# Attention with a top-32 mask, then two expert layers: transposes and v products moved seven and eight heads behind the scores

## The reference, cut to what matters

```python
# attention: B=2, H=8, S=576, D=64
scores = q @ k.T / 8
mask = scores >= (32nd largest of the row)
attn = softmax(where(mask, scores, -1e9))
x = (attn @ v)                      # rearranged to 1152 tokens x 512
# first expert layer: each token goes to one of 8 experts
e_idx = argmax(x @ w_gate + modality_bias[modality_id]);  gate_w = its probability
x[tokens of e] = gate_w * (relu(x @ w1[e]) @ w2[e])
# second expert layer: all of 4 experts, weighted
out = sum_e p[:, e] * (relu(x @ w1b[e]) @ w2b[e])
```

## Time and profile before

| what | us |
|---|---|
| median of 3 runs | 984.77 (984.18 to 985.72) |
| the profiled execution | 985.48 |
| its span in the profile | 983.7 |
| PE busy | 916.5 (93%) |
| DVE busy | 559.4 (57%) |
| ACT busy | 340.7 (35%) |
| POOL busy | 280.1 (28%) |

### The profile page before, as it was taken

The page is one execution under the profiler, slowest core; times in us unless marked ns, Lnnn a source line. Parts: engine busy times, 40 slices in busy tenths (PEclk is TensorE's granted clock), DMA queues, the critical chain, the costliest instruction groups (busy, mean ns, idle before and its releaser), DMA issues.

```text
span 983.7 us, 13497 instructions
## 1 busy us (share of the span) xinstructions
PE 916.5 (93%) x4849; PEld 770.0 (78%) x4849; DVE 559.4 (57%) x1100; ACT 340.7 (35%) x726; POOL 280.1 (28%) x224
## 2 busy tenths in 40 slices
PE   4799999987799999995699979999999999999998
PEld 4688888876667767762477868998989898989897
DVE  4999999659998989834655152332314231423121
ACT  3545555433445645531645141221202120212010
POOL 7667665434657665611011030000000000000000
PEclk8579999978989999998699989999999999999999
DMA  9120000000412632533962441020202020000001
GB/s 215 57 94 22 1 23 12 12 11 21 173 34 87 214 108 97 187 114 104 330 216 101 152 179 70 1 83 4 86 1 78 9 85 0 0 0 0 32 11 53
DMA packets 49396, 75.63 MB, mean 77 GB/s; under 512 B 24624, under 2 KB 24624, under 8 KB 49328
## 3 DMA queue, kind: packets, MB, share of 16 engines
q1 hardware_dynamic: 42160, 61.09, 18.2%
q0 software_dynamic: 4160, 13.63, 4.3%
q10 hardware_dynamic: 3008, 0.05, 0.2%
HBM read 63.49 MB, written 11.27 MB: 76 GB/s over the span
## 4 chain that ended last, share of the span: by engine, by line
PE 85%; issue 5%; POOL 4%; DVE 4%; DMA 1%; ACT 1%; ACTq 0%; POOLq 0%; DVEq 0%
PE bank L1270 19%; PE bank L1271 18%; PE bank L1272 18%; PE bank L1326 9%; PE bank L1392 5%; PE bank L1367 4%; PE bank L1265 3%; PE bank L1383 3%; PE bank L1297 3%; POOL att L605 2%; PE bank L1295 2%; POOL att L608 1%; DVE w1l L1152 1%; DMA x_tok<-y_a,a_pos_i 1%; PE bank L1338 1%
## 5 line engine op out<-in xcount | busy, mean ns | idle before, releaser
L605 POOL TENSOR_SCALAR att<-sc,top 128x576 f32<-128x576 f32 x70 | 120.8, 1725 | 149.8 <-DVE top L1011 138.0
L1011 DVE MAX8 top<-work 128x8 f32<-128x576 f32 x216 | 152.4, 745 | 0.1
L1270 PE MATMUL bank<-xT,w1h 128*128 128x384 f32 x384 | 129.5, 337 | 5.3 <-DVE w1l L1152 5.3
L1271 PE MATMUL bank<-xT,w1l 128*128 128x384 f32 x384 | 129.1, 336 | 0.0
L1272 PE MATMUL bank<-xT,w1h 128*128 128x384 f32 x384 | 129.0, 336 | 0.0
L1207 DVE SCALAR_TENSOR_TENSOR hT<-bank,hT 128x384 fp32r<-128x384 f32 x96 | 53.0, 557 | 130.8 <-ACT hT L914 127.3
L914 ACT ACTIVATE hT<-bank 128x384 fp32r<-128x384 f32 x96 | 46.9, 492 | 200.9 <-PE bank L1272 200.9
L1326 PE MATMUL bank<-v_one,attT 128*128 128x65 f32 (+3 forms) x800 | 112.8, 282 | 0.6 <-ACT av L738 0.6
L1270 PE MATMUL bank<-w2h,hT 128*128 128x512 f32 x288 | 112.2, 390 | 1.2 <-DVE hT L1207 1.2
L1326 PEld LDWEIGHTS bank<-v_one,attT 128*128 128x128 f32 (+3 forms) x800 | 98.9, 190 | 17.7 <-issue 10.4
L1272 PE MATMUL bank<-w2l,hT 128*128 128x512 f32 x288 | 112.2, 390 | 0.0
(11 more groups left out here) (239 smaller groups left out, 1520.2 us busy)
## 6 DMA issues: line engine op xcount, KB each, us to landing
w_raw<-in_moe_w_dram SPq DMA_DIRECT2D x96, 512.0 KB, 5.9
q_raw<-in_q_dram SPq DMA_DIRECT2D x18, 128.0 KB, 2.7
v_one<-in_v_dram POOLq DMA_DIRECT2D x18, 128.0 KB, 5.5
out_dram<-x_tok SPq DMA_DIRECT2D x9, 256.0 KB, 2.0
k_raw<-in_k_dram SPq DMA_DIRECT2D x8, 256.0 KB, 5.2
y_dram<-zero POOLq DMA_DIRECT2D x2, 1024.0 KB, 6.6
y_dram<-b_ys POOLq DMA_DIRECT2D x7, 256.0 KB
x_dram<-x_cur SPq DMA_DIRECT2D x6, 256.0 KB, 2.8
```

The lines of the kernel that those rows point to most:

```text
L605: nc.gpsimd.tensor_scalar(att[:, g % ATR, :], sc[:, g % RING, :], top8[:, g % RING, 3, 7:8], None, ALU.is_ge).then_inc(keep_made, 1)
L1011: nxt = nc.vector.max(out=top8[:, g % RING, i + 1, :], in_=work[:, j, :])
L1270: nc.tensor.matmul(dst, high_lhs, high_rhs, start=start, stop=False)
L1271: nc.tensor.matmul(dst, low_lhs, high_rhs, start=False, stop=False)
```

## The change

It changes no arithmetic. EXP_LAG, TR_LAG and AV_LAG go from 2, 5, 6 to 3, 7, 8, and `att` gets a fourth slot. `normalise(t)` of tiles 0 to 2 moves from the pair of head 8t + 12 to the pair of head 8t + 10, and their `x_transpose` from step 8t + 17 to 8t + 16; later tiles keep their pair and are transposed in step 8t + 19. `split_q(t + 1)` moves ahead of mask 8t, `round_q` one step earlier. `keep_dense` makes three products instead of four. `ranks`, `sum_tokens` and the first slot stand in steps 34, 37 and 41 instead of 37, 40 and 46, and DVE's chunks of `route` are placed by a finer count. The loop has 82 steps instead of 80.

```diff
-        att = a_mid.take("att", [P, 3, S])
+        att = a_mid.take("att", [P, 4, S])
...
-        RING, EXR, ATR = 8, 4, 3
-        EXP_LAG, TR_LAG, AV_LAG, X_LAG, L_LAG = 2, 5, 6, 17, 18
-        STEPS = (T - 1) * H + AV_LAG + H + 2
-        A_START, A_STEP, SPREAD = 46, 7, 5
+        RING, EXR, ATR = 8, 4, 4
+        EXP_LAG, TR_LAG, AV_LAG = 3, 7, 8
+        STEPS = HEADS + AV_LAG + 2
+        RANKS_AT, TOKENS_AT, A_START, A_STEP, SPREAD = 34, 37, 41, 7, 5
...
+        def x_step(t):
+
+            if t == T - 1:
+                return HEADS + AV_LAG
+            return t * H + (16 if t < GA.tiles else 19)
...
             def beside():
-                yield from clock.until(A_START - 3)
+                yield from clock.until(A_START - 2)
                 pool.wait_ge(x_kept, 16 * TB)
...
             for g in range(HEADS - 2):
+                if g % H == 0 and g // H + 1 < T:
+                    split_q(g // H + 1)
                 mask(g)
...
-                if g % H == 1 and g // H + 1 < T:
-                    split_q(g // H + 1)
...
-                if p % H == 2 and p // H + 1 < T:
+                if p % H == 1 and p // H + 1 < T:
                     round_q(p // H + 1)
...
             def beside():
-                yield from clock.until((GA.tiles - 1) * H + L_LAG + 1)
-                yield from route(GA, clock.until((GA.tiles - 1) * H + L_LAG + 4), clock.until((GA.tiles - 1) * H + L_LAG + 8))
+                yield from clock.until(RANKS_AT - 4.5)
+                yield from route(GA, clock.until(RANKS_AT - 3.4), clock.until(TOKENS_AT - 3.6))
...
-                if g0 >= H + 4 and (g0 - H - 4) % H == 0:
-                    between = normalise((g0 - H - 4) // H)
+                for t in range(T - 1):
+                    if g0 == t * H + (10 if t < GA.tiles else 12):
+                        between = normalise(t)
...
-                for i in range(4):
+                for i in range(3):
                     moving = v_one[0][:, i, 0:KC - 1, :].rearrange("p c w -> p (c w)")
...
-                    if p == (GA.tiles - 1) * H + L_LAG + 3:
+                    if p == RANKS_AT:
                         ranks(GA)
-                    elif p == (GA.tiles - 1) * H + L_LAG + 6:
+                    elif p == TOKENS_AT:
                         sum_tokens(GA)
```

More of the change, by code:

```diff
@@ L219, in q_at, with x_at, logits_at @@
             return t if r == 4 and t < T else None, t if r == 5 and t < T else None
[L221 to L226, removed]
+        def x_step(t):
+            if t == T - 1:
+                return HEADS + AV_LAG
+            return t * H + (16 if t < GA.tiles else 19)
+        def x_at(p):
+            return next((t for t in range(T) if x_step(t) == p), None)
+        def logits_at(p):
+            return x_at(p - 1)
         turn_use = {}
@@ L240, in attention_and_experts @@
                 next_use("ql", low)
[L241 to L244, removed]
+            if x_at(p) is not None:
+                next_use("x", x_at(p))
+            if logits_at(p) is not None:
+                next_use("lg", logits_at(p))
         AV_END = HEADS + AV_LAG - 1
@@ L511, in _ @@
                 clock.now = p
-                if x_at(p, X_LAG) is not None:
-                    keep_x(x_at(p, X_LAG))
+                if x_at(p) is not None:
+                    keep_x(x_at(p))
                 low = q_at(p)[1]
@@ L772, in beside @@
             def beside():
-                yield from clock.until(A_START - 8)
+                yield from clock.until(RANKS_AT + 2)
                 act.wait_ge(GA.lsub_made, 1)
@@ L831, in _ @@
                     read_q(low, "ql", qTl, mixed_l)
-                if x_at(p, X_LAG) is not None:
-                    read_x(x_at(p, X_LAG))
+                if x_at(p) is not None:
+                    read_x(x_at(p))
                 if 0 <= p - TR_LAG < HEADS:
@@ L839, in _ @@
                     key_high(SPLIT - 1 + p)
-                if x_at(p, L_LAG) is not None:
-                    read_logits(x_at(p, L_LAG))
+                if logits_at(p) is not None:
+                    read_logits(logits_at(p))
                 advance(work_beside)
@@ L992, in find_thresholds, with pause @@
                 pair = (g0, g0 + 1)
+                def pause():
+                    advance(work_beside)
+                    clock.now += 1 / 7
+                clock.now = g0
                 for g in pair:
@@ L997, in find_thresholds @@
                     nc.vector.max(out=top8[:, g % RING, 0, :], in_=sc[:, g % RING, :]).then_inc(max_found, 1)
-                    advance(work_beside)
+                    pause()
                 k0 = g0 * 5
@@ L1068, in route @@
                 step(nc.vector.tensor_scalar(g.counts[:, 1, :], g.counts[:, 0, :], 0.0, None, ALU.is_gt))
-                yield
                 step(nc.vector.tensor_tensor(g.cmp_pre[:, :, :, :], below[:, :, :].rearrange("p (o e) f -> p o e f", o=1).broadcast_to([P, 2, E + 1, E]),
@@ L1120, in beside @@
             def beside():
-                yield from clock.until((GA.tiles - 1) * H + L_LAG + 1)
-                yield from route(GA, clock.until((GA.tiles - 1) * H + L_LAG + 4), clock.until((GA.tiles - 1) * H + L_LAG + 8))
+                yield from clock.until(RANKS_AT - 4.5)
+                yield from route(GA, clock.until(RANKS_AT - 3.4), clock.until(TOKENS_AT - 3.6))
             work_beside = beside()
             for g0 in range(0, HEADS, 2):
-                clock.now = g0 + 4
                 between = ()
-                if g0 >= H + 4 and (g0 - H - 4) % H == 0:
-                    between = normalise((g0 - H - 4) // H)
+                for t in range(T - 1):
+                    if g0 == t * H + (10 if t < GA.tiles else 12):
+                        between = normalise(t)
                 find_thresholds(g0, between, work_beside)
@@ L1407, in beside @@
                     else:
-                        keep_dense(MB + 2 if p < (GA.tiles - 1) * H + L_LAG + 6 else MB)
+                        keep_dense(MB + 2 if p < TOKENS_AT else MB)
                 for s in range(SPREAD):
@@ L1510, in _ @@
                     q_transposes(low, "ql")
-                if x_at(p, X_LAG) is not None:
-                    x_transpose(x_at(p, X_LAG))
+                if x_at(p) is not None:
+                    x_transpose(x_at(p))
                 if 2 <= p < 2 + T - 1 - SPLIT:
@@ L1521, in _ @@
                     transpose_att(p - TR_LAG)
-                if x_at(p, L_LAG) is not None:
-                    x_logits(x_at(p, L_LAG))
+                if logits_at(p) is not None:
+                    x_logits(logits_at(p))
                 advance(work_beside)
```

## The result

The changed kernel takes 993.09 us (median of 3 runs, 992.48 to 996.31) against 984.77: ratio 1.0092, 95% interval [1.0056, 1.0128]. It is 8.3 us slower. The forecast was 987.0 with a range of 962 to 1003. The profiled execution took 992.48 us, its span is 990.7 (before 983.7).

A forecast was written before the change was run, and what follows sets the result against it. PE and DVE were taken to march side by side without room, PE slower during the slots. The last v product 11.2 us later, less 9.0 of tail, turned 985.48 into 987.7 profiled, 987.0 median; range 962 to 1003.

The forecast's parts named there:

- Slower, by this mechanism: Tiles 0 to 2: den waits for the v product (5.5, 7.2 us), PE idles for x_cur, then half clock; chance 0.45.
- The start, and the fewer products: First heads: PE may lead DVE by about four heads; each step 0.46 us shorter, counting only as lead.
- The first slot: Step 39: gather 2.9 us after head 36's pair starts, landing 4.1, PE idle about 8; head 41's scores copied at 254.6.
- The slots: 30 steps to head 71 at 5.39 are 161.8 us, plus 5 for double products and half clock: 421.5.
- The last steps: Steps 71 to 79: four at 4.8, rest of 71, four bare of about 3: 33 us, last v product at 454.6.
- The tail: Last v product to group b's slot: 7 to 11 us saved from 35.6, taken as 9.
- The sum: Whole kernel: 985.48 + 11.2 - 9.0 = 987.7 us for the profiled execution, median 987.0.
- The lead is already there: Rival, tile 0: head 7's v product copied by 76.1, so DVE never waits; 967 us, chance 0.27.
- The clock stays down: Rival: PE stays longer at half clock, per tile and around step 34, costing 10 to 20 us: 1002; chance 0.16.
- No shorter tail: Rival, after the last heads: SP's loads or b's gather are held by something else; 996 us, chance 0.12.

The follow-up runs named there:

- the combined version: Changed kernel with gather and split_q two masks earlier, tiles 0-2 normalised at 8t + 12, 3-7 at 8t + 14, steps 37, 40, 44: 952.19 us, ratio 0.9674.

## Why the prediction was right or wrong

**Slower, by this mechanism: right, and shown.** `den` of tiles 0 to 2 waits 7.21, 6.63 and 5.84 us (predicted 5.5, 7.2, and a repeat); PE waits 5.20, 5.19 and 4.39 for `x_cur` (4 to 5), then runs at half clock for 8 to 10 us. That last part had luck in it: of the five profiles with these waits and three unread products, four have a stretch of 27 us behind one of them, and this one has none. The pair of head 36 starts at 236.27 (236.1). Taking the early place back from two of three tiles gives back 12 us, and the lags without it, with the old steps, gain 15.5.

**The start, and the fewer products: right.** The clock rose at 47 us, within the first unread products (from 45.29 on), though there are three. They cost nothing, but I gave them no value of their own; alone they are worth 6 us in the kernel before and 3.4 here.

**The first slot: a term mis-sized by 3.8 us.** I let the gather start 2.9 us after its pair and land in 4.1. It started 239.16 - 236.27 = 2.9 after it, but PE began only at 246.93, 7.8 us after the issue; the longest landing of the five gathers was 7.7. The earlier trace rows had a maximum of 7.0 and I took the median. PE at once regained 1.6 of it: 9.9 us, not 11.5, to the scores of head 41 (256.84 against my 254.6).

**The slots: right in sum, in part by luck.** Predicted 166.9 us from head 41 to head 71, measured 167.1. I had added 5 us for tile 4's double products and for first steps at half clock. But the clock was full from 256 us on. The first seven steps took 298.18 - 256.84 = 41.3 us, the next seven, the same steps of the next slot, 336.61 - 298.18 = 38.4, so the double products are worth some 2.9 (an estimate). The rest, about 2.5, is that 5.39 is too little a step for these thirty: the three slots after the first took (412.71 - 298.18) / 3 = 38.2 each, 37.7 by 5.39, and the two steps left over 5.6 each. PE hides the later tiles' `den` waits of 10.23, 5.81, 4.54 and 3.75 us, as said: without them the same stretch takes 166.4.

**The last steps: a term mis-sized by 2.1 us.** From head 71 to the last `den` I had 33.1 us, four bare steps of 3 among them; it took 459.19 - 423.97 = 35.2. The clock falls before the last two of these steps, which hold v products and transposes:

```profile
447.98 1.44 PE L1334 MATMUL bank<-v_one,attT 128*128 128x65 f32 x10 [0.25 <-ACT av L743]
...
451.53 2.56 PE L1334 MATMUL bank<-v_one,attT 128*128 128x65 f32 x10 [1.04 <-ACT av L743]
...
456.34 2.56 PE L1334 MATMUL bank<-v_one,attT 128*128 128x65 f32 x10 [1.04 <-ACT av L743]
```

Ten products take 2.56 us instead of 1.44. Before the clock fell, at about 450.5, PE was busy for 6.84 of the 7.10 us from 443.4 on; the gap of 1.04 us comes at the fall itself. With the slots over in step 75, the lag of eight leaves four such steps where six would leave two.

**The tail: right.** 26.0 us against 26.6 predicted and 35.6 before. SP's weight loads start 472.01 - 459.19 = 12.8 us after the last `den`, 16.9 before, the 4 us earlier of the prediction. Of the 9.6 us the old start step gives back 4.1, the rest stays.

**The sum.** 2.2 (first slot) + 0.2 (slots) + 2.1 (last steps) - 0.6 (tail) + 0.8 (after it, which I had left out) are 4.7 of the 4.8 us between 987.7 and the profiled 992.48; another 1.3 is that I put the median below the profiled run and it lies above.

**The rivals.** *The lead is already there* did not happen, but its premise is true for the longer lag: with `den` at its old place PE is never late for tiles 0 to 3. What was missing was one pair of heads. *The clock stays down* happened in the profiles of four variants, for 27 us at a time, all with three unread products; the one profile with these waits and four has no such stretch. So the reason given may hold, and is not tested: there is one profile of each kernel. What the runs do show is that the fourth product costs 3.4 us net all the same. The Trainium skill ("TensorE: Matmul & The Clock Gate", Part 4: PE-mode transpose) would have given 1002 us; here the early stretch at 0.50 ended with the first unread products at 47 us, three of them being enough, and the time was 993. In the kernel with tiles 0 and 1 normalised later, with the same code up to there, it ended only at 56 us, so once the rise did take a step more, as this rival had it. The last bare steps, all v products and transposes, do fall to half clock, in line with it, though a gap of 1.04 us stands at that place too. *No shorter tail* is out.

## What to carry to other kernels

A longer lag between two engines pays only if what consumes the late result does not move ahead at the same time: keep the reader of the delayed value in its place or move it later, before anything else, and ask what each engine's next in-order wait is. Two engines in lockstep pay a lateness twice, once in idle time and once in PE's clock, so the repairs of one chain should be tried together: three that gave 17 us singly gave 30 in one kernel. Where runs spread by more than an edit is worth, read its worth from the stretch of the profile that it changes, and look whether the stretch ahead of it was the same. Padding that holds the clock has a price, which shows where PE needs a lead, not in the plain steps: three products let the clock fall for 15 us once and were still 5.7 us faster than four.

## What was unexpected of the hardware

Around the same 5.2 us of idle PE half clock lasted 9.9 us in one execution and 27 in another, with the same instructions behind it (PE busy for 25.65 of the 27.00 us). The long stretch stands in the profiles of four variants. Three of them (gather earlier, tiles 3 to 7 later, `split_q` earlier), then the three waits with four unread products, and last the combined version, same columns:

```profile
89.20:116.20 27.00, 25.20 (x88) 20.75 (x89) 27.00 (x56) 9.18 (x23) 18.20 (x12) 0.51 0.03 11
...
89.20:116.20 27.00, 25.89 (x92) 21.48 (x93) 27.00 (x56) 9.18 (x23) 18.65 (x13) 0.50 0.03 11
...
128.90:156.10 27.20, 25.70 (x90) 21.25 (x91) 27.20 (x57) 9.19 (x23) 19.98 (x13) 0.50 0.03 10
...
87.80:94.60 6.80, 5.98 (x23) 5.45 (x24) 6.80 (x15) 3.37 (x9) 5.71 (x4) 0.51 0.10 39
134.00:142.20 8.20, 5.37 (x22) 4.95 (x23) 8.20 (x16) 2.79 (x8) 6.24 (x4) 0.60 0.08 32
182.60:192.20 9.60, 7.38 (x27) 6.46 (x27) 9.60 (x20) 3.73 (x9) 6.24 (x4) 0.54 0.07 27
...
96.80:112.20 15.40, 15.40 (x57) 12.90 (x56) 15.40 (x31) 5.59 (x15) 9.28 (x7) 0.50 0.00 1
```

The last line stands behind no more than 1.83 us of idle, and PE was busy all through it. Such stretches are likely why variants with these waits spread from run to run (980.76 to 995.43; 984.6 to 996.82), while the kernel before stays within 980.92 and 987.91. It is not shown, with one profile for each, but the mean granted clock goes along: in the ten runs with the gather earlier it is 0.929 and 0.930 in the two fastest and 0.919 in the slowest. What decides between 10 and 27 us was not found.

Of five gathers of 128 rows each the quickest landed after 3.4 us and the slowest after 7.7; the slow one was the one that PE waited for.
